# Splitting v 1 on GpSimd instead of ScalarE and VectorE in the opening of a fused attention and MoE kernel

## What is computed

```python
scores = scale * q @ k.T + bias            # 2 x 8 heads, 768 x 768, head size 64
keep = is_global | is_local                # first n_global keys, or the last n_local ones
a = softmax(where(keep, scores, -1e9))
x = (a @ v)                                # to 1536 tokens x 512
h = x @ w_in                               # 512 x 2048
x2 = (h * tanh(softplus(h))) @ w_out       # 2048 x 512
out = sum over e of p[e] * (relu(x2 @ w1[e]) @ w2[e])    # 4 experts, 512 x 1024 x 512
```

## Time and profile before

| | |
|---|---|
| median of 3 runs | 903.66 us |
| the profiled execution, its own time | 902.35 us |
| its span | 900.5 us |
| TensorE busy | 873.6 us (97%) |
| VectorE busy | 483.3 us (54%) |
| ScalarE busy | 319.2 us (35%) |
| GpSimd busy | 257.6 us (29%) |

### The profile page before, as it was taken

The page is one execution under the profiler, slowest core; times in us unless marked ns, Lnnn a source line. Parts: engine busy times, 40 slices in busy tenths (PEclk is TensorE's granted clock), DMA queues, the critical chain, the costliest instruction groups (busy, mean ns, idle before and its releaser), DMA issues.

```text
span 900.5 us, 12637 instructions
## 1 busy us (share of the span) xinstructions
PE 873.6 (97%) x4916; PEld 444.9 (49%) x4916; DVE 483.3 (54%) x1010; ACT 319.2 (35%) x597; POOL 257.6 (29%) x218
## 2 busy tenths in 40 slices
PE   6888999999999999999999999999999999999998
PEld 6666876444444444444444444444444444444443
DVE  7756887999999989874542125222134322212121
ACT  4898886545555656552021110102010111101020
POOL 1278993222222222210029200077000292000000
PEclk9987999999999999999999999999999999999999
DMA  9871420000000000202000500001300000000001
GB/s 214 276 237 37 142 84 1 1 1 1 1 7 3 1 1 1 97 1 94 10 1 0 186 1 1 6 0 53 134 1 6 0 0 0 1 24 23 35 12 49
DMA packets 52004, 39.19 MB, mean 44 GB/s; under 512 B 40816, under 2 KB 41712, under 8 KB 51440
## 3 DMA queue, kind: packets, MB, share of 16 engines
q1 hardware_dynamic: 49888, 34.31, 12.5%
q10 hardware_dynamic: 2064, 4.19, 1.3%
HBM read 35.35 MB, written 3.15 MB: 43 GB/s over the span
## 4 chain that ended last, share of the span: by engine, by line
PE 89%; ACT 5%; DVE 4%; issue 1%; POOL 0%; DVEq 0%
PE bank L607 67%; PE bank L676 14%; PE bank L546 2%; PE bank L578 2%; ACT scaled L865 2%; PE bank L597 2%; ACT tmp L849 1%; ACT tmp L890 1%; PE bank L501 1%; DVE xT L1213 1%; PE bank L559 1%; DVE tmp L1117 1%; ACT hid L839 0%; DVE tmp L1228 0%; DVE tmp L1346 0%
## 5 line engine op out<-in xcount | busy, mean ns | idle before, releaser
L961 ACT ACTIVATE hid<-bank 128x512 f16<-128x512 f32 x96 | 57.3, 597 | 422.2 <-PE bank L607 422.2
L607 PE MATMUL bank<-xT,wA 128*128 128x512 f16 (+1 forms) x864 | 194.6, 379 | 0.0
L1337 DVE SCALAR_TENSOR_TENSOR hid<-bank,hid 128x512 f16<-128x512 f32 x96 | 66.4, 691 | 181.8 <-ACT hid L961 181.8
L607 PEld LDWEIGHTS bank<-xT,wA 128*128 128x128 f16 x864 | 84.5, 98 | 100.6
L676 PE MATMUL bank<-hid,wB 128*128 128x512 f16 x576 | 132.2, 379 | 0.9 <-DVE xT L1213 0.9
L607 PE MATMUL bank<-xT,wB 128*128 x576 | 125.3, 379 | 0.0
L607 PE MATMUL bank<-wA,hid 128*128 128x512 f16 x576 | 125.3, 379 | 0.0
L607 PE MATMUL bank<-wB,hid 128*128 128x512 f16 x576 | 125.3, 379 | 0.0
L815 POOL TENSOR_TENSOR tmp<-tmp 128x512 f32<-128x512 f32 x48 | 61.4, 1280 | 190.2 <-DVE tmp L1360 190.2
L770 POOL TENSOR_SCALAR stage<-stage,sc 128x1024 f32<-128x1024 f32 x32 | 36.0, 1124 | 256.7 <-DVEq L1330 250.4
L1417 DVE SCALAR_TENSOR_TENSOR acc<-bank,pg,acc 128x512 f32<-128x512 f32 x36 | 27.0, 750 | 131.7 <-PE bank L607 131.7
(11 more groups left out here) (111 smaller groups left out, 948.8 us busy)
## 6 DMA issues: line engine op xcount, KB each, us to landing
stage<-in_moe_w SPq DMA_DIRECT2D x8, 2048.0 KB, 9.8
stage<-in_moe_w_in SPq DMA_DIRECT2D x1, 4096.0 KB, 16.6
wB<-in_moe_w_out ACTq DMA_DIRECT2D x1, 4096.0 KB, 16.3
hid<-in_q SPq DMA_DIRECT2D x16, 192.0 KB, 3.4
hid<-in_k SPq DMA_DIRECT2D x16, 192.0 KB, 3.5
xT<-in_v SPq DMA_DIRECT2D x8, 384.0 KB, 5.0
out_y<-acc SPq DMA_DIRECT2D x12, 256.0 KB, 2.0
rows<-max SPq DMA_DIRECT2D x4, 128.0 KB, 4.1
```

What stands on the lines that cost most here:

```text
L607: last = pe.matmul(dst, lhs(c, a), rhs(c, b), start=(c == 0 and n == 0), stop=(c == chunks - 1 and n == 2))
L961: act.activation(hv[:, f, 0, :], psum(f % 4), ACT.Relu).then_inc(f_hi, 1)
L1337: dve.scalar_tensor_tensor(hv[:, f, 1, :], psum(f % 4), 0.0, hv[:, f, 0, :], ALU.max, ALU.subtract).then_inc(f_ready, 1)
```

## The change

GpSimd splits v 1 as well. Its loop now goes on to the split for n = 1; for this piece it waits for `v_scale` 2 (the scale is made) and `v_split` 1 (piece 0 is done), and the numbers of its own semaphore `v_part` move by 3. ScalarE's `values_high(1)` after unit 8 of pair 0 and VectorE's `values_low(1)` after unit 9 are gone. The waits of TensorE are as before.

```diff
@@ GpSimd
                     pool.partition_all_reduce(scale_cols(col)[0], part[:, 4:5] if n else vpart[:, 0:1], P,
                                               ABSMAX).then_inc(v_amax, 1)
+                if n == 0:
                     continue
+                if n == 1:
+                    pool.wait_ge(v_scale, 2)
                 src, hi, lo, ones, zeros = v_pieces(n)
                 pool.wait_ge(v_split, n)
                 pool.tensor_scalar(src, src, scale_cols(col)[2], 1.0, ALU.mult, ALU.mult).then_inc(v_part, 1)
-                pool.wait_ge(v_part, 3 * n - 5)
+                pool.wait_ge(v_part, 3 * n - 2)
                 pool.tensor_scalar(hi, src, 1.0, 1.0, ALU.mult, ALU.mult).then_inc(v_part, 1)
-                pool.wait_ge(v_part, 3 * n - 4)
+                pool.wait_ge(v_part, 3 * n - 1)
                 pool.tensor_tensor(lo, src, hi, ALU.subtract).then_inc(v_part, 1)
-                pool.wait_ge(v_part, 3 * n - 3)
+                pool.wait_ge(v_part, 3 * n)
                 pool.memset(ones, 1.0)
                 pool.memset(zeros, 0.0).then_inc(v_split, 1)
@@ ScalarE
-            def values_high(n):
+            def values_high():
 
-                act.wait_ge(v_scale, n + 1)
-                src, hi = v_pieces(n)[0:2]
-                if n:
-                    act.wait_ge(v_split, n)
-                act.activation(hi, src, ACT.Copy, scale=scale_cols(v_col(n))[2]).then_inc(v_hi, 1)
+                act.wait_ge(v_scale, 1)
+                src, hi = v_pieces(0)[0:2]
+                act.activation(hi, src, ACT.Copy, scale=scale_cols(SC_V0)[2]).then_inc(v_hi, 1)
...
-                    if before(i, slot) is None and u == PAIRS:
-                        values_high(1)
@@ VectorE
-            def values_low(n):
+            def values_low():
 
-                dve.wait_ge(v_hi, n + 1)
-                src, hi, lo, ones, zeros = v_pieces(n)
-                dve.scalar_tensor_tensor(lo, src, scale_cols(v_col(n))[2], hi, ALU.mult, ALU.subtract
+                dve.wait_ge(v_hi, 1)
+                src, hi, lo, ones, zeros = v_pieces(0)
+                dve.scalar_tensor_tensor(lo, src, scale_cols(SC_V0)[2], hi, ALU.mult, ALU.subtract
                                          ).then_inc(v_low, 1)
...
-                elif u == PAIRS + 1:
-                    values_low(1)
```

More of the change, by code:

```diff
@@ L879, in first @@
                     expo(0, 0, 1, banded)
-                values_high(0)
+                values_high()
             def pair(i, slot, banded):
@@ L1181, in matrix_step @@
                         matrix_scale(n, col)
-            def values_low(n):
-                dve.wait_ge(v_hi, n + 1)
-                src, hi, lo, ones, zeros = v_pieces(n)
-                dve.scalar_tensor_tensor(lo, src, scale_cols(v_col(n))[2], hi, ALU.mult, ALU.subtract
+            def values_low():
+                dve.wait_ge(v_hi, 1)
+                src, hi, lo, ones, zeros = v_pieces(0)
+                dve.scalar_tensor_tensor(lo, src, scale_cols(SC_V0)[2], hi, ALU.mult, ALU.subtract
                                          ).then_inc(v_low, 1)
-                dve.wait_ge(v_low, n + 1)
+                dve.wait_ge(v_low, 1)
                 dve.memset(ones, 1.0)
@@ L1258, in attention @@
                 value_step(0)
-                values_low(0)
+                values_low()
                 pair(0, 0, is_banded, lambda u: u and value_step(u))
```

## The result

The changed kernel takes **910.43 us** (median of 6 runs, 909.7 to 912.16); the kernel before, on the same chip, 903.31 us (6 runs, 902.48 to 904.01). The ratio is 1.0081, with a 95% interval of 1.0068 to 1.0094: slower by 7.1 us, clear of the noise though under 1%. The forecast was 912.4, within 907.5 to 914.5. The profiled execution took 912.16 us, the longest of the six; its span is 910.3 us, 9.8 more than in the profile before.

A forecast was written before the change was run, and what follows sets the result against it. TensorE was taken to set the pace from 33 to 46 us, ScalarE from 46 to 62, TensorE gapless from 170. 6.47 for the wait plus 2.3 for the clock, +8.8 on 903.66, gave 912.4 us, range 907.5 to 914.5.

The forecast's parts named there:

- When the new code is there: GpSimd's code is fetched from the change of library on, whatever the engine waits for; v 1's split starts at 39.51.
- the first fetch: GpSimd's code after the library change at 3.6: at most 9.3 us, against 11.2 for the second, which shares full DMA engines.
- the second reading: Rival: GpSimd's fetch comes with the first instruction using the code, behind its wait, some 6 us; 908.0 us, chance 0.19.
- Part 1: Work taken off ScalarE and VectorE: ScalarE's piece brings nothing, VectorE's lets TensorE reach v 1's product 0.91 us earlier, at 35.97.
- Part 2: Added on GpSimd: v 1's split takes 3.77 us, until 43.28; v 2 to 7 move by one split, w_in's stays covered.
- part 3: TensorE's new wait for v 1 leaves it 7.4 us idle, until 43.35: +6.47 us, with nothing caught up after.
- Part 4: TensorE's clock stays at half for 4 to 6.5 us after the long wait: +2.3 us, bounds 0 and 3.5.
- The sum: New wait plus low clock on TensorE: +8.8 us, giving 911.1 from the profiled execution and 912.4 from the median.
- The fetch behind the wait: Rival: GpSimd fetches its code only after its wait, starts at 35.53; some +4.3 us, 908.0 us, chance 0.19.
- hidden: Rival: TensorE's stop falls on slack later, so the end does not move; 903.7 us, chance 0.02.
- faster: Rival: GpSimd starts before 32.1, so v 1 is ready when TensorE comes; -0.9 us, 902.8 us, chance 0.05.

The follow-up runs named there:

- e1: The kernel before, with GpSimd's first split (v 2) held back until the 18th group of products with v; 903.77 us in one run.
- e2: The changed kernel, with the load of w_in held back until piece 1 of v is split; 907.29 us in one run.
- e9: The kernel before, with the second scale's reduction on TensorE and VectorE, GpSimd making the high half of v 1, VectorE the low; 902.47 us, ratio 0.9986.
- e5: The kernel before, with the second scale's reduction on TensorE and VectorE, ScalarE and VectorE still splitting v 1; 904.96 us, ratio 1.0009.
- e6: The kernel of e4 (changed kernel, second scale's reduction on TensorE and VectorE) run again; 902.49 us, ratio 0.998.
- e7: The changed kernel run again without further edits; 911.13 us (4 runs), ratio 1.0078.
- e3: The changed kernel, with 22 unit-matrix matmuls on TensorE ahead of its wait for v 1; 909.48 us, ratio 1.0066.
- e8: The kernel before run again without edits, for a second profile; its span is 903.0 us, 2.5 us longer than in the first.
- e10: The kernel before, with the second scale's reduction on TensorE and VectorE, ScalarE making the high half of v 1, GpSimd the low; 903.25 us, ratio 0.9994.
- e4: The changed kernel, with the second scale's reduction on TensorE and VectorE, so GpSimd changes its library right behind its first reduction; 902.34 us, ratio 0.9982.

## Why the prediction was right, point by point

**When the new code is there: right.** The start at 39.51 was taken over unchanged; it was 40.60 and 39.47 in the two profiles. e1 shows that the fetch runs beside the wait, e2 (one profile) that the load of w_in stretches it. The forecast's argument from the company of the first fetch was weak, though: that one, over in at most 9.3 us, also ran beside full DMA engines, with a share of 1.12 in the kernel before:

```profile
3.60:13.00 9.40, 8.48 (x51) 7.72 (x52) 6.37 (x18) 2.50 (x6) 0.08 (x2) 1.00 1.12 252
```

So the share alone does not say how long a fetch takes; what sets it beyond e2's finding is open. The rule of the Trainium skill, GPSIMD Engine Reference, section 2.1, gives about 6 us with the wait on an event taken off. For the length of a fetch that has the DMA engines nearly to itself e2's trace agrees roughly (6.72 us). That the first call pays it behind its wait, as the second reading had it, e1 contradicts.

**Part 1, wrong on ScalarE's piece: 0.91 us forecast, 1.94 measured at the bias and 1.7 at TensorE.** "ScalarE's piece ends as the transposes that it waits for next do, so nothing comes of it" was wrong. I took the transposes at 30.48 for those that ScalarE needed next; it needed the ones before, long finished. VectorE then waits for ScalarE, as this row of the kernel before says, which the forecast passed over:

```profile
31.43 0.56 DVE L1228 SCALAR_TENSOR_TENSOR tmp<-bank,tmp 128x384 f16<-128x384 f32 x1 [0.83 <-ACT tmp L890]
```

e9 shows ScalarE's piece on the path with 0.85 us, and from e5 to e6 both pieces move the bias by 1.94. At the product with v 1, where the forecast had TensorE at 35.97, it came to its wait at 35.19 in e7 (43.48 less 8.29), 1.7 us ahead of 36.88. In the changed kernel's time this made no difference, as the wait for GpSimd begins earlier and ends at the same time: that the miss did not show is luck.

**Part 2 and part 3: right.** Split of 3.75 us (forecast 3.77), the signal to TensorE 0.25 (forecast 0.07); seven pieces behind each other, none of the later ones waited for; delay 6.60 and 7.72 us (forecast 6.47), nothing caught up later.

**Part 4: right.** 2.1 us in both profiles (forecast 2.3), half clock for some 5.5 us behind the wait. In e3's profile most of the idleness is gone, and with it the half clock and the 2.1.

**The sum against the median: 1.7 us too much.** I added 8.8 us to the median, 903.66, though they came from a profile of 902.35. That execution happened to have no half-clock stretch between 24 us and the product, and e8 shows what one costs there, 2.5 us. The runs of before lean to two clusters: of the 23 beside e9 and e10, 9 lie from 902.3 to 903.1 and 14 from 904.2 to 906.2, but in other sets some lie between (903.74 and 903.81 among the 17 beside e1). That the clock makes the difference is shown for the two profiles and not for the rest: the mean granted clock of a whole run does not sort them (of those 17, 902.63 us has 0.986 and 905.06 has 0.990). In the changed kernel TensorE waits for GpSimd in any case, so what is lost ahead of the wait does not add to the end: in its first profile it was at half clock until about 33 (the score products at 29.98 take 0.80 us for 0.49) and this cost nothing. Added to the profile's own time the sum is 911.1, and the two medians were 910.43 and 911.13. The profiled execution alone, at 912.16, is above it, mainly because GpSimd began 1.1 us later than at 39.51.

**The rivals.** The fetch behind the wait and "hidden" did not happen. Nor did "faster" in the changed kernel. It came out in e4, another kernel that meets its condition: GpSimd began at 29.70, before 32.1. It gained 1.5 us where the forecast had 0.9, which fits a part 1 that was too small.

## What to carry to other kernels

Before work goes to GpSimd, look at what stood idle ahead of its first instruction of that kind: in these traces a change of library left an idle time with no releaser behind it, and the end of it was the earliest start, whatever the semaphores said. Put the change of library early, where nobody waits, and not beside a large load; here one reduction moved to TensorE turned +0.8% into -0.2%, each against the kernel before. And when a new wait is priced, count from a profile and not from a median, since the wait swallows whatever scatter lies ahead of it; and take more than one profile, as the one used here was among the faster executions.

## What was not expected of the hardware

The fetch of GpSimd's code takes longer beside the load of w_in: 6.72 us beside little traffic (one profile), 10.4 to 12.2 us (starts from 38.54 to 40.60) with 4 MB in flight (five profiles). And TensorE's clock drops in some executions of one and the same program and not in others, in the opening where it has gaps: 0.50 or 1.00 between 32 and 38 us, for 2.5 us of the end. Of the six other profiles in which TensorE does not wait for GpSimd, e5, e9 and e10 are at half clock from 34 to 36 us, e1 partly (0.63), e4 not, and e6 (1.00) only before that, from 32 to 34 (0.53).
